# One loop body per expert, y stored by slot and gathered per token, fewer weights beside attention

## The reference, cut to what matters

```python
skip_score = x @ w_skip
do_compute = skip_score > 0
out = x.copy()
xc = x[do_compute]
logits = xc @ w_gate
e_idx = np.argmax(logits, axis=1)
...
gate_w = probs[np.arange(len(xc)), e_idx]
for e in range(E):                      # 8 experts
    mask = e_idx == e
    h = np.maximum(xc[mask] @ w1[e], 0.0)        # 512 x 1024
    y[mask] = gate_w[mask, None] * (h @ w2[e])   # 1024 x 512
out[do_compute] = xc + y
...
h = x @ w_in                            # 512 x 2048
g = h * np.cos(h)
return (g @ w_out).astype(np.float32)
```

## Time and profile before

| | us |
|---|---|
| median of 3 runs | 553.16 (549.69 to 557.82) |
| profiled execution | 549.4, its span 547.6 |
| attention's last values to the slot list | 108.5 to 128.0 |
| first tile's transposes | 136.2 |
| last matmul of the experts | ends 249.2 |
| first product of the dense stage | 267.7 |

### The profile page before, as it was taken

How to read it: one execution, slowest core, us unless ns; L and a number is a source line. 1 busy time by engine, 2 the same in 40 slices (tenths; PEclk the granted TensorE clock), 3 DMA queues, 4 the chain that set the end, 5 groups by cost and what they waited for, 6 DMA issues and landing times.

```text
span 547.6 us, 11031 instructions
## 1 busy us (share of the span) xinstructions
PE 472.2 (86%) x4193; PEld 374.2 (68%) x4193; DVE 288.5 (53%) x715; ACT 228.1 (42%) x554; POOL 112.7 (21%) x179
## 2 busy tenths in 40 slices
PE   2888777565698997949788989999999999999996
PEld 1766665455475664639566768888888888888885
DVE  7786554334000000630478886667767666657574
ACT  1685555420232442310455544445454445444443
POOL 6585333203424221322303320000000000000000
PEclk9998888955898998988799999999999999999999
DMA  9999999959999928981500000006000001000002
GB/s 213 243 270 270 261 259 299 258 173 405 356 303 408 368 79 294 345 313 42 210 0 1 0 2 0 1 1 229 2 1 1 1 0 65 13 0 1 1 1 77
DMA packets 38687, 78.93 MB, mean 144 GB/s; under 512 B 4656, under 2 KB 18224, under 8 KB 38640
## 3 DMA queue, kind: packets, MB, share of 16 engines
q1 hardware_dynamic: 35984, 71.46, 42.3%
q0 software_dynamic: 1760, 4.98, 2.7%
q10 hardware_dynamic: 896, 1.84, 1.1%
HBM read 65.95 MB, written 10.75 MB: 140 GB/s over the span
## 4 chain that ended last, share of the span: by engine, by line
PE 41%; DVE 7%; ACT 3%; issue 2%; DMA 1%; POOL 0%; POOLq 0%; DVEq 0%; ACTq 0%
PE bank L1130 13%; PE bank L1132 13%; PE bank L1131 13%; DVE turns L973 3%; DVE reduced L977 1%; DVE reduced L980 1%; ACT turns L695 1%; PE bank L1230 1%; DVE reduced L983 1%; DMA y_stage<-y_tokens 1%; DVE gT_lo L992 0%; ACT wout_hi L676 0%; ACT turns L702 0%; DMA y_tokens<-y_out,row_of_slot_now 0%; ACT h_copy L698 0%
## 5 line engine op out<-in xcount | busy, mean ns | idle before, releaser
L1130 PE MATMUL bank<-wout_hi,gT_hi 128*128 128x512 f32 x192 | 75.8, 395 | 7.1 <-DVE gT_lo L992 7.1
L1130 PE MATMUL bank<-x2T,win_hi 128*128 128x512 f32 x192 | 76.3, 397 | 1.4 <-DVE x2T L960 1.4
L1132 PE MATMUL bank<-x2T,win_lo 128*128 128x512 f32 x192 | 75.3, 392 | 0.0
L1131 PE MATMUL bank<-x2T,win_hi 128*128 128x512 f32 x192 | 75.2, 392 | 0.0
L1132 PE MATMUL bank<-wout_hi,gT_lo 128*128 128x512 f32 x192 | 74.9, 390 | 0.0
L1131 PE MATMUL bank<-wout_lo,gT_hi 128*128 128x512 f32 x192 | 74.8, 390 | 0.0
L702 ACT ACTIVATE turns<-reduced,half_pi 128x512 f32<-128x512 f32 x48 | 34.7, 724 | 82.3 <-DVE reduced L983 82.3
L973 DVE TENSOR_SCALAR turns<-turns 128x512 f32<-128x512 f32 x48 | 31.3, 652 | 61.0 <-ACT turns L695 61.0
L695 ACT ACTIVATE turns<-bank,quarter 128x512 f32<-128x512 f32 x48 | 33.0, 686 | 61.6 <-PE bank L1132 61.6
L934 DVE CAST win_hi<-w_slot 128x1024 fp32r<-128x1024 f32 x8 | 5.6, 705 | 91.6 <-DMA w_slot<-weights 91.6
L1130 PEld LDWEIGHTS bank<-wout_hi,gT_hi 128*128 128x128 f32 x192 | 36.0, 188 | 18.3 <-DVE gT_lo L992 10.9
(11 more groups left out here) (157 smaller groups left out, 753.9 us busy)
## 6 DMA issues: line engine op xcount, KB each, us to landing
w_slot<-weights SPq DMA_DIRECT2D x80, 512.0 KB, 7.0
k_padded<-k_T SPq DMA_DIRECT2D x8, 384.0 KB, 9.0
v_tok<-v_pairs SPq DMA_DIRECT2D x8, 384.0 KB, 10.5
v_window<-v_pairs SPq DMA_DIRECT2D x8, 384.0 KB, 10.8
y_tokens<-zeros SPq DMA_DIRECT2D x6, 512.0 KB, 11.2
x_tile<-x_plain SPq DMA_DIRECT2D x12, 256.0 KB, 4.7
out<-out_stage SPq DMA_DIRECT2D x12, 256.0 KB, 2.1
q_blockdiag<-q_T SPq DMA_DIRECT2D x12, 192.0 KB, 10.7
```

Of the source, the lines that this page charges most:

```text
L1130: te.matmul(out_ap, a[0], b[0], start=start, stop=False)
L1131: te.matmul(out_ap, a[0], b[1], start=False, stop=False)
L1132: return te.matmul(out_ap, a[1], b[0], start=False, stop=stop)
```

## The change

PE has one body for each expert, a loop over its tiles from the first to the last, with both products of a tile in it. The second product is in two halves, by the two transposed parts of the hidden values, each copied by ACT on its own, in two PSUM banks. ACT stores y of a tile itself, with a direct DMA at an offset that follows the tile number, into a table of slots; the store waits for that of the tile before. When all are stored, POOL gathers the y of each token by its slot (`slot`; a token that isn't computed has a row of zeros, `ZROW`), 12 gathers in place of 12 loads. `idx4` and all that makes it are gone. The table takes 7 stores of zeros in place of 6. Beside attention 8 chunks of weights are issued in place of 15; those left of experts 0 and 1, and expert 2, wait for the second chunk before them instead of the fourth, and experts 3 and 4 wait until 4 blocks of x are there. The loads of `vtok` come later in SP's order, the first block means (`make_summary(1)`, `sum_tokens(0)`, `copy_vs(0, 1)`) later on DVE and PE, and one of three zeroings of `qbd` moves from DVE to POOL. 24 products instead of 46 keep PE busy before the dense stage. Also left out of this print: deleted constants of `idx4` on POOL (`spread4`, `spare`, `group_col`), its five DVE steps and its product on PE.

```diff
+ZROW = MAXT * MT
+ZSTORES = -(-(ZROW + 1) // (2 * P))
...
-WARM = (4, 46)
-BESIDE = (1, 2, 2, 2, 2, 2, 2, 2)
+WARM = (4, 24)
+BESIDE = (0, 1, 1, 1, 1, 1, 1, 2)
...
-        def weights_wait(eng, e, half):
-            for c in range(NCH // 2 * half, NCH // 2 * (half + 1)):
+        def weights_wait(eng, e):
+            for c in range(NCH - FLIGHT, NCH):
                 chunk_wait(eng, SLOT_OF[e], e // SLOTS, c)
...
-            def load_chunk(src, s, c, load=0):
-                if c >= FLIGHT:
-                    chunk_wait(sp, s, load, c - FLIGHT)
+            def load_chunk(src, s, c, load=0, flight=FLIGHT):
+                if c >= flight:
+                    chunk_wait(sp, s, load, c - flight)
                 sp.dma_start(wslot[s][:, c, :], weights[NCH * src + c, :, :]).then_inc(w_loaded[s][c % FLIGHT], 16)
...
             place_vsum(0)
+            load_vtok(2)
...
             for i in range(PAIRS):
-                if i + 2 < PAIRS:
-                    load_vtok(i + 2)
                 if i + 3 < PAIRS:
                     load_k(i + 3)
                 if i == 1:
                     sp.wait_ge(zeros_ready, 1)
-                if 1 <= i <= NT // 2:
+                if 1 <= i <= ZSTORES:
                     store_zeros(i - 1)
                 for n in range(sent, sent + BESIDE[i]):
...
                     load_windows(i + 1)
+                    if i + 3 < PAIRS:
+                        load_vtok(i + 3)
                     place_vsum(i + 1)
...
             for n in range(sent, 2 * NCH):
-                load_chunk(n // NCH, n // NCH, n % NCH)
+                load_chunk(n // NCH, n // NCH, n % NCH, 0, 2)
             for gr in range(GPP):
                 store_x(STEPS - GPP + gr + 1, TPB + 2 * gr, TPB + 2 * gr + 2, PPB - 1, PPB)
             sp.wait_ge(xps_ready, STEPS)
-            for e in (2, 3, 4):
+            for c in range(NCH):
+                load_chunk(2, SLOT_OF[2], c, 0, 2)
+            sp.wait_ge(blocks_ready, 4)
+            for e in (3, 4):
...
+            g.memset(qbd[2][0:D, 1, :], 0.0).then_inc(q2_zeroed, 1)
+            pool.wait_ge(identw_ready, 1)
+            pool.wait_ge(zeros_ready, 1)
+            pool.wait_ge(q2_zeroed, 1)
+            g.memset(qbd[2][D:P, 0, :], 0.0).then_inc(q2_zeroed, 1)
+            pool.wait_ge(q2_zeroed, 2)
...
-            pool.wait_ge(base_ready, 2)
-            nblocks = pool.value_load(base[0:1, E + 1:E + 2], min_val=E // CG, max_val=NBLK)
...
-            def scatter_block(k):
-                for j in range(CG):
-                    ge(pool, y_stored[j], 16 * k)
-                    g.tensor_copy(idx_now[:, j:j + 1], idx4[:, bass.ds(k, 1), j:j + 1].rearrange("p o q -> p (o q)"))\
-                        .then_inc(idx_copied, 1)
-                    if not isinstance(k, int):
-                        pool.sem_inc(y_free, 1)
-                    pool.wait_ge(idx_copied, CG * k + (j + 1))
-                    primed(pool, y_copied, CG * k + (j + 1))
-                    pool.sem_inc(y_taken, 1)
-                    pool.indirect_dma_start(yd, bass.IndirectOffsetOnAxis(ap=idx_now[:, j:j + 1].bitcast(U32), axis=0),
-                                            y_out[:, j, :], None).then_inc(y_stored[j], 16)
-            scatter_block(0)
-            with pool.Fori(1, nblocks) as k:
-                scatter_block(k)
-            for j in range(CG):
-                pool.wait_ge(y_stored[j], 16 * nblocks)
-            pool.sem_inc(y_all, 1)
...
+            def gather_y(t, q):
+                ge(pool, x2_done, t - (TPG - 1))
+                pool.indirect_dma_start(yst[q][:, :], None, yd,
+                                        bass.IndirectOffsetOnAxis(ap=slot[:, t:t + 1].bitcast(U32), axis=0))\
+                    .then_inc(yst_loaded[q], 16)
+            pool.wait_ge(slot_ready, 1)
+            pool.wait_ge(y_all, 1)
+            for t in range(2 * TPG):
+                gather_y(t, t % TPG)
...
+            for t in range(2 * TPG, NT):
+                gather_y(t, t % TPG)
...
             def copy_y(n):
+                primed(act, y_ready, n + 1)
+                sc.activation(y_out[:, bass.ds(n % CG, 1), :].rearrange("p o f -> p (o f)"), y_ps[:, 0:P], ACT.Copy)\
+                    .then_inc(y_copied, 1)
+            ytiles = yd[0:ZROW, :].rearrange("(n r) (g c) -> n g r c", r=MT, g=CG)
+            def store_y(n):
+                primed(act, y_copied, n + 1)
+                primed(act, y_stored, 16 * n)
+                act.dma_start(ytiles[bass.ds(n, 1), :, :, :].rearrange("n g r c -> (n g) r c"),
+                              y_out[:, bass.ds(n % CG, 1), :].rearrange("p o f -> p (o f)")).then_inc(y_stored, 16)
+            def copy_hT(n, j):
+                primed(act, t2_ready[j], n + 1)
                 primed(act, y_ready, n)
...
-                act.wait_ge(y_free, n)
-                sc.activation(y_out[:, bass.ds((n - 1) % CG, 1), :].rearrange("p o f -> p (o f)"), y_ps[:, 0:P], ACT.Copy)\
-                    .then_inc(y_copied, 1)
-            def copy_hT(n):
-                primed(act, t2_ready, n + 1)
-                primed(act, y_ready, n)
-                sc.activation(hT[:, :, :], ht_ps[:, 0:JC * P].rearrange("p (j q) -> p j q", j=JC), ACT.Copy)\
-                    .then_inc(ht_ready, 1)
+                sc.activation(hT[:, j, :], ht_ps[j][:, 0:P], ACT.Copy).then_inc(ht_ready[j], 1)
...
             copy_xT(0)
-            copy_block(1)
-            relu(0)
-            copy_xT(1)
-            copy_hT(0)
-            with act.Fori(1, ntiles) as n:
+            act.wait_ge(zero_stored, 16 * ZSTORES)
+            with act.Fori(0, ntiles) as n:
                 copy_block(n + 1)
                 relu(n)
+                for j in range(JC):
+                    copy_hT(n, j)
                 copy_xT(n + 1)
                 copy_y(n)
-                copy_hT(n)
-            copy_y(ntiles)
-            primed(act, y_copied, ntiles)
-            act.sem_inc(y_copied, CG - 1)
+                store_y(n)
+            primed(act, y_stored, 16 * ntiles)
+            act.sem_inc(y_all, 1)
...
-                act.dma_start(yst[q][:, :], src).then_inc(yst_loaded[q], 16)
...
-            for s in range(3):
+            for s in range(2):
...
-            make_summary(1)
-            sum_tokens(0)
             for s in range(STEPS):
                 neg_scores(s, s % GPP, s % 2)
                 if s == 0:
+                    make_summary(1)
+                if s == 1:
+                    sum_tokens(0)
+                if s == 2:
                     copy_vs(0, 1)
...
+            v.tensor_scalar(slot[:, :], rank[:, :], float(ZROW), None, ALU.min).then_inc(slot_ready, 1)
...
             for s in range(STEPS):
                 scores(s)
-                if s == 0:
+                if s == 2:
                     pe.wait_ge(ident_ready, 1)
                     sum_values(0, 1)
...
             def second_product(n, e):
-                primed(pe, ht_ready, n)
-                primed(pe, y_copied, n - 1)
+                primed(pe, y_copied, n)
                 w = wslot[SLOT_OF[e]]
-                for k in range(CG * JC):
-                    for g in range(CG):
-                        o = DM * (k % 2) + P * g
-                        last = te.matmul(y_ps[MT * g:MT * (g + 1), 0:P], hT[:, k % JC, MT * (k // JC):MT * (k // JC + 1)],
-                                         w[:, KC + k // 2, o:o + P], start=(k == 0), stop=(k == CG * JC - 1))
+                for j in range(JC):
+                    primed(pe, ht_ready[j], n + 1)
+                    for k in range(j, CG * JC, JC):
+                        for g in range(CG):
+                            o = DM * (k % 2) + P * g
+                            last = te.matmul(y_ps[MT * g:MT * (g + 1), 0:P], hT[:, j, MT * (k // JC):MT * (k // JC + 1)],
+                                             w[:, KC + k // 2, o:o + P], start=(k == 0), stop=(k == CG * JC - 1))
                 last.then_inc(y_ready, 1)
...
-            def tile(n, e, behind):
+            def tile(n, e):
                 first_product(n, e)
                 transpose_block(n + 1)
-                if behind is not None:
-                    second_product(n, behind)
-                    if behind != e:
-                        expert_read()
                 primed(pe, relu_done, n + 1)
-                primed(pe, ht_ready, n)
                 for j in range(JC):
-                    last = te.transpose(ht_ps[:, P * j:P * (j + 1)], hid[:, P * j:P * (j + 1)], ident[:, :])
-                last.then_inc(t2_ready, 1)
+                    te.transpose(ht_ps[j][:, 0:P], hid[:, P * j:P * (j + 1)], ident[:, :]).then_inc(t2_ready[j], 1)
+                second_product(n, e)
...
             for e in range(E):
-                weights_wait(pe, e, 0)
-                tile(first[e], e, e - 1 if e else None)
-                weights_wait(pe, e, 1)
-                with pe.If(first[e] + 1 < first[e + 1]):
```

(13 more changed lines are left out.)

68 lines of the change are left out of this document (18 added, 50 removed).

## The result

The changed kernel takes 573.46 us (median of 4 runs, 570.82 to 574.83) against 551.42 of the kernel before (median of 4, 546.49 to 557.82): a ratio of 1.0425, 95% interval 1.0333 to 1.0516. It is slower. The execution that the profile shows has a span of 573.1 us, 25.5 more than before, and the first dense product comes 25.4 us later, at 293.07 for 267.69. So all of the loss lies ahead of the dense stage, as the prediction assumed, but with the other sign.

A forecast was written before the change was run, and what follows sets the result against it. Attention was taken as DMA-bound, the expert stage as PE time with 28 us of gaps. First transposes -7.3, expert stage -7.9 and tail -4.4 gave -19.6 from 549.4: 529.8, scaled to 533 us; range 519 to 549.

The forecast's parts named there:

- the tile, 18 x 5.5 = 99.0: Expert stage: 18 tiles at 5.5 us each, priced by a scatter's landing; part of a stage of 105.1 us against 113.0.
- that just fits: Expert stage: ACT's other work, 1.9 us, fits under the next tile's first product, 1.93 us.
- The store's landing sets the tile: Rival, expert stage: ACT's wait for the previous y store adds up to 41 us, 574 in all; chance 0.05.
- Attention: Attention stage: seven fewer chunks save 9.5 us, less 2 for a start gap; its end moves by -7.5 us.
- The 2 us for the start: Start of attention: later first block means hold back SP's DMAs, a gap of 0 to 4 us, taken as 2.
- The x stores: Routing: the last three stores of x, now behind eight chunks, delay the first gather to 123.0, +1.5 us.
- Fetches: Expert stage on PE: of 15.8 us idle for instruction fetches, 1 us stays; bounds 0 and 15.8.
- Fetches stay: Rival, expert stage: instruction packets still come late while weights stream, 14.8 us return, 548; chance 0.15.
- loops fetch anew: Rival, expert stage: each jump back in PE's loops fetches its code again, 30 us, 563; chance 0.03.
- The tail: From last expert product to first dense product: 14.0 us against 18.4, -4.4; bounds -7 and 0.
- first-byte latencies: Expert stage: page estimate, the store lands 0.4 us sooner, tile 5.15, sum 6 us lower; weighed, 5.5 taken.

The follow-up runs named there:

- e2: The changed kernel with no store of y at all; 527.92 us.
- e6: The changed kernel with ACT storing only 32 of the 128 partitions of each y; 540.66 us.
- e7: The changed kernel with y scattered by POOL's indirect DMA, four buffers, and the last three x stores behind three chunks instead of eight; 531.58 us, ratio to before 0.9626.
- e10: e7 with only 6 of 14 blocks of x gathered at once, the other 8 only above 23 tiles; 523.35 us, ratio to before 0.9529.
- e9: The changed kernel with the first block means early again and the `vtok` loads before the keys; 581.36 us.
- e5: The changed kernel with 15 chunks of weights beside attention again; 578.87 us.
- e12: e7 with a second, never entered loop per expert on PE, to be jumped over; 545.12 us, ratio to before 0.9932.
- e1: The changed kernel with y stored by POOL instead of ACT, plain DMA, four buffers; 562.74 us, ratio to before 1.0216.
- e11: The changed kernel with two chunks of weights in flight everywhere instead of four; 560.22 us.

## Why the prediction was wrong

**The step that failed is the tile, 18 x 5.5 = 99.0, and in it first the landing of the store.** "The nearest price is the scatter's: 5.4 loaded ... I take 5.5 per tile; bounds 5.2 and 6.3 as a mean." The same bytes were taken to be the same transfer. They aren't: the scatter puts 64 KB into some 32 packets, ACT's store into some 130 of 512 B, and beside the weights that takes 6.7 to 9.8 us, the first 16.4. The stage came to 145.1 us, 8.1 per tile, where 105.1 was said. e2 prices the stores in all (46.9 us of span); 24 of them are waits for landings. e6 shows that with a quarter of the partitions (4.9 us to land) all but five landings leave the path.

**The second error in that step: "that just fits."** ACT's work from y's copy to the relu was summed to 1.9 us against 1.93. It is 2.39, and 2.12 with the small store of e6. The issue itself was priced high, 0.59 for 0.7; what was mis-sized are the gaps, 0.32 us before it and 0.67 behind it, for 0.24 in all. So even a store that lands at once makes a tile 5.63 (e6) or 5.91 (after) for e2's 4.97, 12 to 17 us in all. The tile's own path was over-priced, 5.15 for 4.97.

The rival "The store's landing sets the tile" had the right number, 574, partly by luck. It has every tile wait for a landing of 7.8, and 18 x 2.3 = 41 us. In the trace eight stores wait for nothing and one landing takes 16.4, and ACT's own path, which the rival doesn't have, makes up the difference. It got 0.05 because its price was capped by "the worst landing seen, 7.8", the worst of another kind of transfer. A bound taken from a row of another operation isn't a bound.

**Attention: right at the row predicted, and more behind it.** -7.5 was said for the values that wait for the last means, -7.6 was measured (108.51 to 100.94); with the spread of single runs, that it fits to 0.1 is luck. The prediction called those "the last values", but two more steps follow. Before, PE came to them out of a wait of 5.86 us and had a granted clock of 0.50 of full speed (1.2 GHz), 1.12 us for 16 matmuls; after, it had waited 0.33 us and had 1.00 (2.4 GHz), 0.69 us. So the slot list gained 11.8. In e7 and e10 these two steps take 1.12 us again, so the 4.2 us beyond the 7.6 aren't sure. The 2 us for the start aren't shown (e9), and seven chunks are worth 10.9 (e5), not 9.5.

**The x stores: +1.5 said, +9.9 measured.** A gather follows the slot list by 1.04 us, so 117.3 would have been free; it was 127.17. The issue came when it was said: 123.0 less "some 2 us" for the stores is 121.0, and SP issued the first at 120.99. The stores' own landing was mis-sized: the gather followed 6.2 us behind that issue, and the last store, issued at 121.98, took 4.9 of them. The median of the three is 3.7 us; before, it was 2.0. That is 4.2 us of the miss, the same kind of error as with y. The other 4.2 is that the list was ready 4.3 us sooner than thought, with nothing gained by it. Then errors cancelled: gather to transposes took 4.6 for the 5.8 said, and the first transposes stand at 131.77 for 128.9.

**Fetches: right.** 15.8 to 1.7, said 1, and the 1.7 lie in the first tile. "Fetches stay" and "loops fetch anew" are excluded, the first by the profile and e12.

**The tail: half.** -2.2 for -4.4. The dense product follows the last product by 16.2 in place of 14.0.

Put together, the rest of the change is worth about what was forecast: e7, which keeps the single bodies, the gathers and the fewer chunks, but scatters y from POOL and stores x earlier, is at 0.9626, and took 531.6 where 533 was said. That it fits so well is luck. Its first transposes come 3.4 us sooner than said, its stage has tiles of 4.97 for 5.5 but a wait of 8.9 for POOL, and its tail is 20.6 for 14.0. The kernel as changed lies 24 us above the range's upper end, 549.

**What stays open.** e6 takes away packets and bytes together. That it is the packets, not the bytes, rests on e7's equal bytes in 32 packets, and on the landings beside the weights: 4.8 to 7.1 us for 32 packets and 64 KB (e7), 3.9 to 6.1 for 48 and 16 KB (e6, behind the third), 4.9 to 7.3 for 80 and 64 KB (e1), 6.7 to 9.8 for 132 and 64 KB (after). The bytes set no order among them. But in e1 a plain store by POOL is 80 packets, of which 64 are under 512 B, so the bytes lie in the other 16 (on empty queues two such stores took 2.9 and 3.0 us). How much belongs to the size of the packets that carry the bytes and how much to their count or to the queue wasn't separated: no run sends the same packets by both. e11 shows that the weights in flight count too, but not how. Nor is it shown why the first store took 16.4.

## What to carry to other kernels

Price a DMA by a row with the same packet sizes and the same queue, not by one with the same bytes, and ask what streams beside it. A wait for a landing belongs on an engine with nothing behind it, and with as many buffers as the landing is tiles long; on an engine that feeds the bottleneck it holds up the tile, and even a landing that is over in time costs its issue and the gaps around it. When a list of waits names a DMA, look whether the next issue came late: of 51.7 us here, 24 were the landing's. When an early stage is sped up, look at once for what the next stage waits for besides: here three small stores behind eight chunks took 9.9 of the 11.8 us, and a change of SP's order got 5 to 10 back.

## What the runs showed of the hardware that wasn't expected

A store of 130 packets of 512 B has passed 2.1 us after its issue when the queues are empty, and takes 6.7 to 9.8 beside the weights, though it is an eighth of one chunk in bytes. With two chunks in flight instead of four, ACT's wait for it falls from 24.1 to 10.9 us (e11). While it runs, the trace counts 114 packets of weights for 27 of the store's in a microsecond (166 to 167 us), about four to one, over 16 engines.

The page "DMA: Bandwidth & Descriptors" of the Trainium skill (Queues, rings and completion order) says that each DMA engine takes turns between the queue rows for which it has work, a packet at a time. The trace agrees that a store shares the engines and isn't served first. By the same section such a packet holds several descriptors, so it need not be what the trace counts as one, and the four to one measured doesn't test whether the turns are even. By an estimate from that page's first-byte latencies (Specifications), which the prediction weighed, the store would have landed 0.4 us sooner than a scatter; on empty queues 2.1 us against the scatter's 2.3 doesn't speak against that, but beside the weights it landed 1.3 to 4.4 later (6.7 to 9.8 against the scatter's median of 5.4), so there those latencies aren't what decides.

Code that is never run cost 13.8 us of span (e12), by being jumped over while weights stream: 10.4 us of it are gaps in which PE waits, with 13 packets of instructions for seven.
